# Eight steps' weights made in place, unit 0 scored first, and the sums of x moved into weight set 3

## Time and profile before

| | |
|---|---|
| median of three runs | 1144.32 us |
| profiled execution | 1145.91 us |
| its span | 1143.9 us |
| TensorE (PE) busy | 1098.1 us, 96% |
| VectorE (DVE) busy | 822.1 us, 72% |
| ScalarE (ACT) busy | 781.3 us, 68% |
| GpSimd (POOL) busy | 389.7 us, 34% |
| HBM traffic | 302.8 MB through the queues, 265 GB/s |

### The profile page before, as it was taken

One profiled execution on the slowest core, in us unless ns is written; L12 is line 12 of the kernel. 1 busy time (PEld: TensorE's weight loads), 2 busy tenths in 40 slices (PEclk: granted clock), 3 DMA queues, 4 the chain that ended last, 5 costly groups with the idle time before them and its releaser, 6 DMA issues.

```text
span 1143.9 us, 18152 instructions
## 1 busy us (share of the span) xinstructions
PE 1098.1 (96%) x5787; PEld 876.1 (77%) x5787; DVE 822.1 (72%) x1210; ACT 781.3 (68%) x1842; POOL 389.7 (34%) x427
## 2 busy tenths in 40 slices
PE   8999898979999999989999999999999999999998
PEld 4667666757767778878788787888888888888886
DVE  5796686458886965898877968868848568576475
ACT  4797686667658757758758678667677476774574
POOL 5789689741232432136276113663000000000000
PEclk9999999989999999999999999999999999999999
DMA  9998999989889989869899789898697666776664
GB/s 202 268 273 254 345 330 354 348 268 323 251 237 251 269 256 263 280 210 348 301 358 348 233 263 373 300 349 282 186 282 233 189 198 189 219 218 193 194 192 158
DMA packets 204054, 302.80 MB, mean 265 GB/s; under 512 B 112824, under 2 KB 121016, under 8 KB 203960
## 3 DMA queue, kind: packets, MB, share of 16 engines
q1 hardware_dynamic: 203960, 301.65, 85.4%
HBM read 226.10 MB, written 75.50 MB: 264 GB/s over the span
## 4 chain that ended last, share of the span: by engine, by line
PE 73%; ACT 6%; DMA 6%; DVE 5%; issue 4%; POOL 3%; SPq 3%; ACTq 0%; POOLq 0%; DVEq 0%
PE ps L1020 35%; PE ps L1005 31%; DMA w_scratch<-w_new 3%; ACT ps L1100 2%; PE ps L914 2%; DMA w_ring<-w_scratch 1%; DVE g_lo L1494 1%; PE ps L939 1%; POOL w_new L801 1%; PE ps L966 1%; POOL att L801 1%; ACT elu L1193 1%; PE ps L923 1%; PE ps L908 1%; DVE nbias L1347 1%
## 5 line engine op out<-in xcount | busy, mean ns | idle before, releaser
L1005 PE MATMUL ps<-xc_hi,w_ring 128*128 128x512 f32 x1344 | 435.9, 397 | 5.0 <-ACT s L1166 3.7
L1020 PE MATMUL ps<-g_hi,w_ring 128*128 128x512 f32 x1344 | 420.4, 394 | 11.4 <-issue 6.4
L1005 PEld LDWEIGHTS ps<-xc_hi,w_ring 128*128 128x128 f32 x1344 | 253.9, 189 | 63.8 <-issue 4.0
L1020 PEld LDWEIGHTS ps<-g_hi,w_ring 128*128 128x128 f32 x1344 | 249.9, 189 | 68.3 <-issue 9.0
L1005 PE MATMUL ps<-xc_lo,w_ring 128*128 128x512 f32 x672 | 263.2, 392 | 0.0
L1020 PE MATMUL ps<-g_lo,w_ring 128*128 128x512 f32 x672 | 263.1, 392 | 0.0
L801 POOL TENSOR_TENSOR w_new<-w_raw,w_new 128x256 fp32r<-128x256 f32 x179 | 165.9, 933 | 219.0 <-ACT w_new L1247 215.8
L1494 DVE TENSOR_TENSOR g_lo<-X,g_hi 128x512 fp32r<-128x512 f32 x240 | 178.4, 748 | 30.5 <-ACT g_hi L1233 30.0
L1233 ACT ACTIVATE g_hi<-X 128x512 fp32r<-128x512 f32 x240 | 150.1, 629 | 56.8 <-PE ps L1020 55.1
L1020 PEld LDWEIGHTS ps<-g_lo,w_ring 128*128 128x128 f32 x672 | 126.7, 189 | 26.9
L1005 PEld LDWEIGHTS ps<-xc_lo,w_ring 128*128 128x128 f32 x672 | 127.2, 189 | 24.4
(11 more groups left out here) (125 smaller groups left out, 1350.5 us busy)
## 6 DMA issues: line engine op xcount, KB each, us to landing
w_ring<-w_scratch SPq DMA_DIRECT2D x336, 512.0 KB, 4.4
w_scratch<-w_new SPq DMA_DIRECT2D x179, 256.0 KB, 5.3
w_scratch<-att SPq DMA_DIRECT2D x45, 256.0 KB, 4.8
w_raw<-in_moe_w_in SPq DMA_DIRECT2D x16, 512.0 KB, 5.6
w_raw<-in_moe_w_out SPq DMA_DIRECT2D x16, 512.0 KB, 6.0
x_scratch<-y SPq DMA_DIRECT2D x12, 512.0 KB, 6.1
att<-x_scratch SPq DMA_DIRECT2D x12, 512.0 KB, 5.9
out<-elu SPq DMA_DIRECT2D x24, 256.0 KB, 4.3
```

Source lines behind the costliest of these rows:

```text
L1005: last = nc.tensor.matmul(bank_of(st, st.i), w[:, a, cols], x[:, st.pi, kk, :], start=(st.pi in (P1, P5) and kk == 0 and n == 0), stop=(kk ...
L1020: last = nc.tensor.matmul(bank_of(st, d), w[:, a, cols], x[:, k % RING, :], start=(st.pi in (P1, P5) + (P4,) * (1 - st.gr) and st.i == 0 a ...
```

## The change

- **Weights in the ring.** The eight products that steps 0 to 7 use (pp 0, 7, 4, 11, 5, 12, 3, 10 in the order of the steps) are made directly in the four slots of `w_ring`. Steps 0 to 7 wait for GpSimd's low part instead of a load. The loads d = 0 to 3 are gone. The eight are still saved to DRAM, for tiles 1 and 2, and load d = 4 to 7 waits for the saves of the two that stand in its slot.
- **Order of saves.** `SAVE_ORDER`: the first 16 products that are not in the ring, then the eight of the ring, then the rest. Three saves stand in the loads of units 0 to 8 (before: 10), `2 * it + 2` are out behind iteration it, at most 24; the 25th follows the head; the rest two per load. The sets of raw weights follow their saves.
- **Slots.** The 27 products below 35 that are not in the ring take the four slots of `w_new` in turn. Products 35, 36 and 37 take the three slots in `att`, and from there on the seven go round.
- **Unit 0.** q and k of unit n + 1 are loaded ahead of v of unit n. TensorE scores unit 0 and then transposes k and q of unit 1.
- **Sums of x.** The first group is made behind P7 of set 3, the second behind P2 of set 3.

```diff
-HEAD_SAVES = 32
+HEAD_SAVES = 25
...
+def ring_step(pp):
+    m, pi = PREP[pp]
+    g = up_step(0, 0, 0, pi, m)
+    return g if m < 2 and g < 2 * W_RING else None
+
+HEAD_MADE = [pp for pp in range(HEAD_PREP) if ring_step(pp) is None]
+RING_MADE = sorted((pp for pp in range(HEAD_PREP) if ring_step(pp) is not None), key=ring_step)
+HEAD_OWN = HEAD_MADE.index(PREP_AT[3, P2])
+SAVE_ORDER = HEAD_MADE[:HEAD_OWN] + RING_MADE + HEAD_MADE[HEAD_OWN:] + list(range(HEAD_PREP, 2 * PRODUCTS))
...
         def w_slot(pp):
+            if pp < HEAD_PREP and ring_step(pp) is not None:
+                return SAVES + 3 + ring_step(pp)
+            if pp < HEAD_PREP:
+                return HEAD_MADE.index(pp) % SAVES
             if HEAD_PREP <= pp < WIDE_END:
-                return (pp - HEAD_PREP) % (SAVES + 3)
+                return (pp - HEAD_PREP + SAVES) % (SAVES + 3)
...
         def w_at(pp):
+            if w_slot(pp) >= SAVES + 3:
+                return w_ring[:, ring_step(pp) // 2, ring_step(pp) % 2]
...
-            def save_weights(pp):
+            def save_weights(number):
+                pp = SAVE_ORDER[number]
...
-                if d >= W_RING:
-                    sp.wait_ge(step_done, 2 * (d - W_RING) + 2)
+                sp.wait_ge(step_done, 2 * (d - W_RING) + 2)
+                if d < 2 * W_RING:
+                    for g in range(2 * (d - W_RING), 2 * (d - W_RING) + 2):
+                        wait_w_saved(sp, RING_MADE[g])
...
             saves = 0
+            load_qk(0)
             for n in range(AHEAD):
-                load_qk(n)
+                if n + 1 < AHEAD:
+                    load_qk(n + 1)
                 load_v(n)
                 if n in (0, 2):
                     load_raw(n // 2)
-                while saves < 2 * (n - 3):
+                while saves < n - 5:
...
-                while saves < min(HEAD_SAVES - 4, 2 * it + 12):
+                while saves < min(HEAD_OWN + 2 * W_RING, 2 * it + (2 if it else 3)):
                     save_weights(saves)
                     saves += 1
-                if 12 <= it < 12 + W_RING:
-                    load_weights(it - 12)
-            save_x0(HEAD - 4)
-            while saves < HEAD_SAVES - 2:
+            while saves < HEAD_SAVES:
                 save_weights(saves)
                 saves += 1
+            save_x0(HEAD - 4)
...
-            for m in range(4):
+            for m in range(3):
                 prepare((m,))
-            sums_of_head(0)
-            sums_of_head(1)
+            prepare((3,), lambda: sums_of_head(0), lambda: sums_of_head(1))
...
-                if g % 2 == 0:
-                    pe.wait_ge(w_in[g // 2 % W_RING], 16 * (g // 2 // W_RING + 1))
+                if g < 2 * W_RING:
+                    pe.wait_ge(w_lo_done, RING_MADE[g] + 1)
+                elif g % 2 == 0:
+                    pe.wait_ge(w_in[g // 2 % W_RING], 16 * (g // 2 // W_RING))
...
-                if 0 <= it + 1 < HEAD:
+                if 0 <= it + 1 < HEAD and it != 0:
                     transpose_q(it + 1)
...
+                if it == 0:
+                    transpose_k(1)
+                    transpose_q(1)
-                if it + 2 < HEAD:
+                if it + 2 < HEAD and it != -1:
                     transpose_k(it + 2)
...
-                if pp == HEAD_PREP + SAVES:
+                if pp == HEAD_PREP:
                     act.wait_ge(pv_done, HEAD)
-                if pp == HEAD_PREP + SAVES + 2:
+                if pp == HEAD_PREP + 2:
                     act.wait_ge(x0_saved[1], 16 * x_uses(HEAD - 1, 1))
```

More of the change, by code:

```diff
@@ L426, in build @@
         w_hi_act = sem("w_hi_act")
-        w_saved = [sem(f"w_saved{i}") for i in range(SAVES + 3)]
+        w_saved = [sem(f"w_saved{i}") for i in range(SAVES + 3 + 2 * W_RING)]
         w_in = [sem(f"w_in{i}") for i in range(W_RING)]
@@ L505, in w_slot @@
         def w_slot(pp):
+            if pp < HEAD_PREP and ring_step(pp) is not None:
+                return SAVES + 3 + ring_step(pp)
+            if pp < HEAD_PREP:
+                return HEAD_MADE.index(pp) % SAVES
             if HEAD_PREP <= pp < WIDE_END:
-                return (pp - HEAD_PREP) % (SAVES + 3)
+                return (pp - HEAD_PREP + SAVES) % (SAVES + 3)
             return pp % SAVES
         slot_uses = []
-        used = [0] * (SAVES + 3)
+        used = [0] * (SAVES + 3 + 2 * W_RING)
         for pp in range(2 * PRODUCTS):
@@ L725, in _ @@
             save_x0(HEAD - 3)
-            while saves < HEAD_SAVES:
-                save_weights(saves)
-                saves += 1
             for d in range(W_RING, STEPS // 2):
@@ L801, in split_w, with prepare @@
                 nc.gpsimd.tensor_tensor(lo, src, hi.bitcast(F32), ALU.subtract).then_inc(w_lo_done, 1)
-            def prepare(ms):
+            def prepare(ms, after_p7=None, after_p2=None):
                 blocks = [tuple(weight_blocks(m)) for m in ms]
@@ L818, in prepare @@
                         split_w(m, pi)
+                    if pi == P7 and after_p7:
+                        after_p7()
+                    if pi == P2 and after_p2:
+                        after_p2()
                 for m, (a11, a12, a21, a22) in zip(ms, blocks):
```

## The result

The changed kernel took 1149.63 us (median of 20 runs, 1145.49 to 1152.69) beside 1143.47 us for the kernel before (20 runs, 1140.2 to 1151.14): a ratio of 1.0043, 95% interval 1.0031 to 1.0056. Timed again on another chip it took 1148.44 beside 1144.84 us, 1.0026 (1.0013 to 1.0039). I had predicted 1139.8 and a range of 1133 to 1148. By the ratios it is 3 to 5 us slower (the medians lie 6.2 and 3.6 us apart), and not 4.5 faster; both ratios lie within the 0.5% that I had called no change.

What follows compares the result with a forecast made beforehand. It took the DMA-full head, then the release behind it, as limits. Head gains 2.2 + 3.6 + 2.1 = 7.9 us shrank to 4.2 at the release; with 0.3 after it, 1144.3 - 4.5 = 1139.8 us, range 1133 to 1148.

Steps and rivals of the forecast that it cites:

- (a): Start of the head: unit 0 scored ahead of unit 1's transposes, near 9.3 us; gain 2.2 us, between 0 and 2.3.
- (b): SyncE's queue in the head: fewer saves ahead of unit 8's loads end its k wait and half clock; gain 3.6 us.
- (c): Late head: sums of x inside weight set 3 end ScalarE's wait for them; gain 2.1 us, between 0 and 3.2.
- T: End of the last PV product of the attention head; forecast at 99.6 us instead of 107.5.
- (d): Ahead of step 0: the four ring loads (2 MB) go; claimed to give nothing itself.
- The second limit: Behind the head: saves and GpSimd's weight set 4 hold ScalarE's cut for product 37 until T + 14.3, bounds 12.5 to 18.
- the release: Start of ScalarE's cut for product 37, ahead of step 10; forecast at 113.9 us instead of 118.1, 4.2 earlier.
- What follows it: Behind the release: loads one further ahead against GpSimd's arrears; gain 0.3 us, ends -1.5 and +1.5.
- A: Rival: the head's whole gain of 7.9 us arrives, release at T + 10.6 or less, 1136 us; chance 0.20.
- B: Rival: the DMA-bound head hardly moves, about 3.5 us, and nothing is left behind it, 1144.5 us; chance 0.18.
- C: Rival: slow landings of saves 25 to 30 put the release at T + 20 or more, 1150 us; chance 0.12.
- the mark: Sign set beforehand for rival C: step 10, behind the head, starts after 119 us.

Runs made afterwards that it cites:

- r4: The kernel before with only unit 0's part of the change (earlier q and k loads, unit 0 scored first): 1145.37 us, ratio 0.9998.
- r13: The changed kernel run again without edits, for its trace: the profiled execution took 1147.89 us.
- r14: The changed kernel run again without edits, for its trace: the profiled execution took 1143.59 us.
- r12: The kernel before with only the sums of x moved inside weight set 3: 1151.30 us, ratio 1.0077.
- r3: The changed kernel with saves 24 to 29 brought forward: 1138.09 us, ratio to the kernel before 0.9942.
- r16: The changed kernel with the third save and raw weights of set 2 issued behind unit 9's q, k and mem_k: 1146.41 us, ratio to the kernel before 1.0013.
- r10: The changed kernel with 29 saves instead of 25 ahead of the loop of loads: 1139.93 us, ratio to the kernel before 0.9970.

## Why the prediction was wrong, by its own steps

**(a) Unit 0, 2.2 us.** Scored 3.2 earlier, unit 2 by 1.8, unit 6 by 2.4. Right in size. Alone it is worth nothing (r4).

**(b) Unit 8's k, 3.6 us.** From unit 6 to unit 8 the lead grows from 2.4 to 6.0, so 3.6 as forecast. But "what is late next is nothing" was wrong: in three of five executions the k of unit 9 was late by 0.7 to 2.0 us, behind the raw weights of set 2, and in r13 the low clock followed.

**(c) Sums of x, 2.1 us of 0 to 3.2.** This term was mis-sized. ScalarE no longer waits for the sums, as predicted, but the lead at unit 16 is 5.6 and at unit 8 it was 6.0: nothing came. The two low parts of x met the second group of sums: 2.92 us for two, TensorE late by 1.14 us at 82.55, and the granted clock 0.72 from 82 to 88 us. I had counted nothing for this because it stood at 3.16 us before; but it now fell on TensorE's path. I should have carried the 1.6 us as a loss that could appear, not as a gain.

The first sum of x came at 71.1, later than the 65 to 70 that I had forecast, the second group at 77.9 as forecast.

So T was 101.9 and not 99.6, and in this trace all of the 2.3 us are (c)'s. In the trace of r14, where VectorE was not held and no k was late, it was 100.2; in that of r13, where the k of unit 9 was 1.99 us late and the low clock followed, 104.0.

**(d)** The ring loads gave nothing, as said; but they were what held r12, so the part was worth nothing only beside the others.

**The second limit, T + 14.3.** This is the step that failed most, beside (c). Its terms, against the trace of after:

| term | predicted | measured |
|---|---|---|
| q, k, mem_k; save 27, raw, save 28; load 6, x, v | 6.5 | 7.2 (109.15 - 101.92) |
| save 29 to its slot taken, product 33 | 3.6 + 1.37 | 5.5 + 1.4 |
| sum, product 34, first sum of set 5 | 2.8 | 2.9 |
| T to the start of the cut | 14.3 | 17.1 |

The structure was right link by link, and T + 17.1 is inside my bounds of 12.5 to 18. The landing was mis-sized: I took 3.6 us from the saves of the head, 0.88 of DMA share in mind, while this save stands behind a raw load of 0.5 MB, unit 17's v and load 6, and took 5.4. Nearer rows stood in the trace of the kernel before, the saves issued from 114 to 160 us among the same kinds of loads:

```profile
DMA to landing us min/median/max: 3.4/5.5/6.6
```

With T 2.3 us and the chain 2.8 us too low the release came at 118.99 and not at 113.9. That is 0.8 later than before, where I had forecast 4.2 earlier.

**What follows it, +0.3 gained.** Not seen. In the first trace the end of step 10 is 0.8 us later than before, of step 12 1.2 and of step 24 1.5; by the end of step 84 (273.7 and 273.8) and of step 112 (325.9 and 326.0) the two kernels are level. Step 10 takes 2.9 us in both traces, so the low clock in it is not new with the change.

**What the steps add up to.** The median of 1149.6 lies 9.8 us above the forecast. About 5 of them are the release, 0.8 later in place of 4.2 earlier: 2.3 from T, 2.8 from the chain. The other 5 or so are in no step of the prediction and not in the first trace either.

**The rivals.** A asked for T + 10.6; r3 shows that it would have come with the saves ahead, at T + 6.7. B gave 1144.5 for a head that hardly moves: the head did move. C is what happened, in its mechanism: T 101.9 where it said 101, landings of 5.4 where it said 6.3, T + 17.1 where it said T + 20 to T + 21; and by the mark I had set (step 10 after 119) it was C, though the mark was a weak one: in the kernel before step 10 started at 119.27. Its 1150 us lie close to the 1149.6 measured, but its release at 122 does not to the 119.0 of the trace, so that closeness is luck as far as the traces show. I gave it 0.12. I should have seen that the threshold of C, T + 18.5, held only for T = 99.6: with T at 101.9 it is T + 16.2, well inside the bounds of the forecast itself. Two terms that I bounded apart decide together.

**What stays open.** The traces put the changed kernel at 1143.6 to 1147.9 us (five) beside one of before at 1145.9; the timed medians put it 3 to 5 us behind. The one trace of before is 2.4 us above the median of its 20 runs, and the first of after 4.1 below its own. r13 shows one way to be late and r16 points the same way; no execution of 1149 us or more was caught with a trace, so for those the place is not shown.

## What to carry to other kernels

When a producer's slots come free through saves that stand in one queue with loads, follow that queue beyond the stretch that is being shortened: if a save waits behind a load that waits for the end of the stretch, the gain can end at the next wait, as it did here. The order of four to six saves was worth 6 to 10 us (r10, r3), and it turned a change that cost 3 to 5 us into one that gains 7. Price a landing from rows with the same neighbours in the queue, and where two uncertain terms add up to a threshold, take the chance of their sum. And try each part alone: of three parts here none gained alone.

## What was not expected of the hardware

**VectorE and GpSimd, whoever comes first.** In the changed kernel the two low parts of x (both inputs in SBUF) beside GpSimd's sums took 2.92 us:

```profile
78.98 2.92 DVE L1399 TENSOR_TENSOR xc_lo<-X,xc_hi 128x512 fp32r<-128x512 f32 x2
```

In r14, the same kernel in another execution, VectorE took 1.28 us for them

```profile
79.52 1.28 DVE L1399 TENSOR_TENSOR xc_lo<-X,xc_hi 128x512 fp32r<-128x512 f32 x2
```

and the sum beside them 2.66 us, where the others take 1.27 to 1.81:

```profile
79.28 2.66 POOL L871 TENSOR_TENSOR X<-X 128x512 f32<-128x512 f32 x1
```

In the first trace both engines lose: VectorE 1.6 us, and three of GpSimd's sums 0.3 to 0.5 us each over the 1.27 of an undisturbed one. In r14 GpSimd alone loses, 1.4 us. So who pays changes between executions of one kernel, and with it goes TensorE's wait at 82.55; step 0 starts at 89.40 and not at 91.12. The Trainium skill says this (SBUF — State Buffer, "SBUF: two separate sides"): of a VectorE operation with two inputs in SBUF and a GpSimd operation that reads SBUF, the one that starts first gets the shared ports for its whole instruction, and the other is blocked. The first trace agrees: GpSimd's sum was running when VectorE's operations started at 78.98. In r14 the recorded starts do not: GpSimd's sum is recorded 0.24 us ahead of VectorE's operations (79.28 and 79.52) and yet it is the one that takes longer. Whether the recorded start is the moment at which the ports are taken, no run here shows.

**A late load can cost more than its wait, and need not.** In r13 the k of unit 9 is 1.99 us late. Up to unit 7 this execution was 1.1 us ahead of r14; unit 9 is scored 3.9 us behind it, so the late load cost 5.0 us. The granted clock from 46 to 56 us was 0.66 against 1.00. In r10 the same load is 1.93 us late, and the clock does not fall:

```profile
47.53 0.66 PE L908 MATMUL ps<-ident,y 128*128 128x128 f32 x4 [1.93 <-DMA y<-in_mem_k]
```

```profile
46.00:56.00 10.00, 8.41 (x97) 6.29 (x98) 7.29 (x11) 8.17 (x38) 7.03 (x10) 1.00 1.03 249
```

There unit 8 is scored 6.6 us behind unit 7, where 4.6 is usual: the wait and nothing more. What decides between the two is not shown. Around the 9.27 us of idle time at step 10 the granted clock was 0.57 in the mean of 112 to 124 us, a window of which the wait itself fills 8 us.
